# Rebuilding the routing and the row fetch of a second expert layer: one table at the end against one token tile at a time

## The chip, the cores and the metric

The kernel runs on one core of a Trainium2 chip. The metric is the device time in microseconds (us). A core has the matrix engine PE, the vector engine DVE, the scalar engine ACT, GpSimd (POOL) and the sync engine SP, each with its own instruction queue taken in order. They meet through semaphores. DMAs are issued from SP, ACT and POOL.

## The reference, cut to what matters

```python
x = _attn_ref(...)             # (1536, 512) after the heads are laid side by side
x = _moe_ref(x, ...)           # every token through all 8 experts, weighted by P
# second expert layer: each token goes to one expert only
xn = x / (norm(x) + 1e-6); en = emb / (norm(emb) + 1e-6)
logits = xn @ en.T / tau
expert_idx = argmax(logits, axis=1)
probs = softmax(logits); gate_w = probs[arange(N), expert_idx]
for e in range(8):
    mask = expert_idx == e
    h = maximum(x[mask] @ w1[e], 0.0)
    out[mask] = gate_w[mask, None] * (h @ w2[e])
```

Sizes: N = 1536 tokens (12 tiles of 128), D = 512, F = 1024. All is float32. A product is made from high and low parts in float32r: `matmul_x3` issues three PE matmuls for one.

## The kernel before

**Stages.** Attention, then expert layer one (`m1`), then expert layer two (`m2`). Layer one goes through 8 experts; each has three chunks `c` of 512 tokens, and each chunk an up phase (8 groups `f` of 12 matmuls, counted by `m1.up`) and a down phase (32 steps `j` of 3 matmuls, `m1.down`), after which DVE adds the expert's output into `tok` (`m1.y`). In the last expert's last chunk the down phase goes tile by tile (`final`), so that the four y additions come one after another.

**Routing of layer two, before.** The x of 512 tokens is turned by PE (`turn_x`), split by ACT and DVE, multiplied with the split embeddings (`gate`, 512 columns wide) and turned back (`turn_gate`). Chunks 0 and 1 are done inside the last expert of layer one, chunk 2 and everything after it when that expert has ended: norms, argmax and softmax for all 12 tiles at once on DVE, two products for the ranks inside a tile, running sums over tiles and experts, and a place for each token. An expert's tokens fill whole tiles of 128 slots. POOL then writes all twelve tiles of `tok` with twelve indirect DMAs (scatters) to `x_sorted` in DRAM. A row there has 514 columns: x, the weight, the token's number + 1. `x_sorted` is cleared beforehand by 21 DMAs of zeros that SP issues during attention. SP reads the two extra columns back (`meta`), and ACT loads a tile's rows with plain DMAs (`load_row`).

**Layer two, before.** For each expert the engines loop over its tiles `i` (`tile_range`, loop bounds from `start_i`). PE: two up halves `c` of 12 matmuls with a turn of the relu's output between them (`turn_h`), the turn of the next tile's rows (`turn_row(i + 1)`), then the down phase of 24 matmuls with a second `turn_h`. ACT writes y of the tile before (`y_tile`) and high parts; DVE does relu and low parts. POOL stores a tile's y with an indirect DMA (`store`), waits until it has landed, and frees `y_row`.

**Weights of layer two, before.** One raw buffer each for w1 and w2, two sets of split buffers (`w1_p`, `w2_p`). ACT makes the high parts of expert e + 2 when expert e is through (`w1_hi2`, `w2_hi2`), DVE the low part of w1 (`w1_lo2`) and half of w2's (`w2_lo2`), POOL the other half of w2's. SP starts a load of 2 MB when the raw buffer has been split.

## Time and profile before

| | us |
|---|---|
| median of 3 runs | 1652.41 (1651.46 to 1652.56) |
| profiled execution, its own time | 1649.05 |
| its span, first to last instruction | 1647.3 |
| PE busy in the span | 1569.6 (95%) |
| DVE, ACT, POOL busy | 609.7, 469.7, 324.4 |
| mean granted clock of PE, share of full speed | 0.978 |

Busy PE is not PE at its peak: matmuls are pipelined, and the time between the starts of two is less than the duration listed for one. Idle time of another engine costs something only where PE, or the end, waits for it. The page's slices show PE at 9 tenths or more through layer one, a hollow at the layer change, and 9 again after it. The profile's line numbers (L391 to L393 are the three matmuls of `matmul_x3`) are those of the functions printed above.

### The profile page before, as it was taken

How to read it: one execution, taken by the hardware profiler on the slowest of the kernel's cores; microseconds unless marked ns; L12 is line 12 of the kernel's file. 1: busy time of each engine (PE TensorE's matmuls, PEld its weight loads, DVE VectorE, ACT ScalarE, POOL GpSimd, SP SyncE). 2: the span in 40 equal slices, each digit the busy share in tenths (PEclk: the TensorE clock that was granted, in tenths of full speed). 3: DMA queues.
4: the chain of work that ended last, by engine and by line, in shares of the span. 5: the costliest groups of instructions: out<-in, count | busy, mean ns of one | idle time of the engine just before them, and what ended most of it. 6: DMA issues, size and time to landing. Idle time of an engine off the chain costs nothing.

```text
span 1647.3 us, 21247 instructions
## 1 busy us (share of the span) xinstructions
PE 1569.6 (95%) x7516; PEld 1309.9 (80%) x7517; DVE 609.7 (37%) x1021; ACT 469.7 (29%) x864; POOL 324.4 (20%) x527
## 2 busy tenths in 40 slices
PE   7999999999999999999999999999999992799998
PEld 6899998788888888888888888888888771577776
DVE  5888888342221211211211322322222234554324
ACT  4777777112111111111111211211111132654113
POOL 4445444100300300210020030030030004332202
PEclk8999999999999999999999999999999995899999
DMA  4665664100100110110110110020020014754310
GB/s 121 177 156 141 157 141 162 52 1 0 69 35 1 62 40 0 51 51 0 51 51 0 51 51 0 0 102 0 0 82 21 0 52 141 262 191 143 132 45 24
DMA packets 50405, 115.94 MB, mean 70 GB/s; under 512 B 7862, under 2 KB 9910, under 8 KB 50368
## 3 DMA queue, kind: packets, MB, share of 16 engines
q1 hardware_dynamic: 44432, 102.39, 20.1%
q10 hardware_dynamic: 3536, 6.75, 1.5%
q0 software_dynamic: 2400, 6.31, 1.0%
q8 instruction: 22, 0.36, 0.1%
q14 instruction: 15, 0.12, 0.0%
HBM read 81.58 MB, written 13.40 MB: 58 GB/s over the span
## 4 chain that ended last, share of the span: by engine, by line
PE 85%; DVE 4%; DMA 3%; issue 3%; POOL 3%; ACT 1%; SPq 1%; DVEq 0%; ACTq 0%; POOLq 0%
PE psum L391 24%; PE psum L393 24%; PE psum L392 24%; PE psum L624 3%; DMA w_raw<-in_moe_w_dram 2%; PE psum L613 2%; PE psum L637 1%; PE psum L638 1%; PE psum L614 1%; PE psum L595 1%; PE psum L829 1%; DVE row_min L1118 1%; PE psum L649 1%; POOL x_sorted L530 1%; DVE pt_lo L1108 1%
## 5 line engine op out<-in xcount | busy, mean ns | idle before, releaser
L976 ACT ACTIVATE h_hi<-psum 128x512 fp32r<-128x512 f32 x192 | 114.9, 599 | 867.5 <-PE psum L393 867.5
L391 PE MATMUL psum<-xt_lo,w_hi 128*128 128x512 f32 x768 | 303.9, 396 | 0.2 <-DVE xt_lo L1213 0.2
L393 PE MATMUL psum<-xt_hi,w_lo 128*128 128x512 f32 x768 | 301.1, 392 | 0.0
L391 PE MATMUL psum<-w_lo,h_hi 128*128 128x512 f32 x768 | 300.0, 391 | 0.0
L393 PE MATMUL psum<-w_hi,h_lo 128*128 128x512 f32 x768 | 299.3, 390 | 0.0
L392 PE MATMUL psum<-w_hi,h_hi 128*128 128x512 f32 x768 | 298.9, 389 | 0.0
L392 PE MATMUL psum<-xt_hi,w_hi 128*128 128x512 f32 x768 | 298.8, 389 | 0.0
L1298 DVE SCALAR_TENSOR_TENSOR h_lo<-psum,h_hi 128x512 fp32r<-128x512 f32 x192 | 132.7, 691 | 360.8 <-ACT h_hi L976 360.7
L424 POOL CAST w_hi<-w_raw 128x512 fp32r<-128x512 f32 x64 | 39.9, 624 | 813.1 <-PE psum L393 803.8
L1341 DVE SCALAR_TENSOR_TENSOR tok<-psum,route,tok 128x512 f32<-128x512 f32 x84 | 57.5, 744 | 384.6 <-PE psum L393 384.6
L393 PEld LDWEIGHTS psum<-xt_hi,w_lo 128*128 128x128 f32 x768 | 144.2, 188 | 33.4
L392 PEld LDWEIGHTS psum<-xt_hi,w_hi 128*128 128x128 f32 x768 | 144.2, 188 | 31.5
L393 PEld LDWEIGHTS psum<-w_hi,h_lo 128*128 128x128 f32 x768 | 144.1, 188 | 30.6
L392 PEld LDWEIGHTS psum<-w_hi,h_hi 128*128 128x128 f32 x768 | 144.2, 188 | 30.3
L391 PEld LDWEIGHTS psum<-xt_lo,w_hi 128*128 128x128 f32 x768 | 144.4, 188 | 29.7 <-DVE xt_lo L1213 0.4
L391 PEld LDWEIGHTS psum<-w_lo,h_hi 128*128 128x128 f32 x768 | 144.2, 188 | 29.9
L1108 DVE TENSOR_TENSOR pt_lo<-psum,pt_hi 128x384 fp32r<-128x384 f32 x192 | 98.1, 552 | 35.8 <-ACT pt_hi L877 33.7
L884 ACT ACTIVATE prob<-psum,row_bias,row_scale 128x768 f32<-128x768 f32 x96 | 96.5, 1006 | 20.3 <-POOL row_bias L468 20.2
L877 ACT CAST pt_hi<-psum 128x384 fp32r<-128x384 f32 x192 | 83.1, 487 | 44.5 <-PE psum L624 44.5
L1118 DVE TENSOR_REDUCE row_min<-psum 128x1 f32<-128x768 f32 x96 | 90.9, 947 | 8.3 <-PE psum L614 8.3
L508 POOL TENSOR_TENSOR w_lo<-w_raw,w_hi 128x512 fp32r<-128x512 f32 x64 | 83.4, 1303 | 12.7 <-issue 7.4
L613 PE MATMUL psum<-k_b,q_b 128*128 128x384 f32 x192 | 75.0, 390 | 8.3 <-DMA q_b<-bits 4.0
(236 smaller groups left out, 1903.5 us busy)
## 6 DMA issues: line engine op xcount, KB each, us to landing
w_raw<-in_moe_w_dram SPq DMA_DIRECT2D x32, 2048.0 KB, 8.3
k_hh<-k_hi SPq DMA_DIRECT2D x32, 192.0 KB, 3.0
x_sorted<-zeros SPq DMA_DIRECT2D x21, 257.0 KB, 3.9
x_row<-x_sorted ACTq DMA_DIRECT2D x19, 256.0 KB
k_raw<-in_k_dram SPq DMA_DIRECT2D x8, 384.0 KB, 3.2
v_raw<-in_v_dram SPq DMA_DIRECT2D x16, 192.0 KB, 3.5
k_b<-k_lo SPq DMA_DIRECT2D x16, 192.0 KB, 3.3
q_raw<-in_q_dram SPq DMA_DIRECT2D x7, 384.0 KB, 3.7
```

The lines of the kernel that those rows point to most:

```text
L391: pe.matmul(acc, a[0], b[1], start=start, stop=False)
L392: pe.matmul(acc, a[0], b[0], start=False, stop=False)
L393: return pe.matmul(acc, a[1], b[0], start=False, stop=stop)
L508: pool.tensor_tensor(w2_s[1][:, f, :], w2_raw[:, f, :], w2_s[0][:, f, :].bitcast(F32), ALU.subtract).then_inc(m1.w2_lo, 1)
L613: pe.matmul(o, q_b[u][:, a], k_b[u][:, b], start=True, stop=False)
L877: act.copy(pt_hi[half][:, 3 * c:3 * c + 3, a:a + P], psum[:, 4 + c, 0:HALF].rearrange("p (j i) -> p j i", j=3)).then_inc((s_hi_a, s_hi_b)[ ...
L884: act.activation(prob[t % 2][:].rearrange("p (c j) i -> p c (j i)", c=2), psum[:, 2 * (t % 2):2 * (t % 2) + 2, 0:HALF], ACT.Exp, bias=row_ ...
L976: act.activation(h_s[0][:, f, :], psum[:, f % 4, :], ACT.Relu).then_inc(m1.h_hi, 1)
L1108: dve.tensor_tensor(pt_lo[half][:, 3 * c:3 * c + 3, a:a + P], psum[:, 4 + c, 0:HALF].rearrange("p (j i) -> p j i", j=3), pt_hi[half][:, 3 ...
L1118: dve.tensor_reduce(row_min[:, c], psum[:, 2 * (t % 2):2 * (t % 2) + 2, 0:HALF], AX.XY, ALU.min).then_inc(s_min, 1)
L1298: dve.scalar_tensor_tensor(h_s[1][:, f, :], psum[:, f % 4, :], 0.0, h_s[0][:, f, :].bitcast(F32), ALU.max, ALU.subtract).then_inc(m1.h_lo, 1)
L1341: dve.scalar_tensor_tensor(tok[:, tile, 0:DM], psum[:, 4 + i, :], route[:, e, tile:tile + 1], tok[:, tile, 0:DM], ALU.mult, ALU.add).then_ ...
```

## The change

**Token tiles.** In the last expert of layer one each token tile t goes through its own routing: PE turns the tile (`turn_token`), ACT copies it and squares the rows (`token`), PE multiplies with the embeddings in plain fp32 (`token_logits`), DVE picks the expert as a one-hot row (`choose`), PE counts the tokens before each one (`token_rank`), DVE makes from the rank a one-hot lane times the token's number and a one-hot cell of expert and block (`find_cell`), PE multiplies the two (`table_part`), and DVE adds the product into a table of (expert, block) by lane (`add_part`). The norm no longer stands ahead of the argmax. Tiles 0 to 3 go beside chunk 1's down phase (`tokens_beside`), 4 to 6 beside chunk 2's up phase, 7 to 10 beside its down phase (`tokens_between`), tile 11 behind it. The gate products, `turn_gate`, the running sums and the 512-wide turns and splits for layer two are gone.

**Rows.** `x_sorted`, its zeros and the twelve scatters are gone. SP stores each tile of `tok` in token order to `x_rows` when it is final, and the softmax weights to `weights`. POOL gathers the rows of a tile with an indirect DMA through the table; the first tile's indices come from a product of their own. In each tile POOL now issues the store, a gather of 128 weights (`p_now`) and the gather of the rows for tile i + 2. ACT's `load_row` is gone.

**Weights.** w1 of experts 0, 1 and 2 is loaded ahead of layer two, the second into the place of the then dead x. w2 has two raw buffers. POOL makes all of w2's low parts and those of w1 for experts 0 and 1; DVE only w1's from expert 2 on. In a tile, the second `turn_h` stands at f = 1, not 2. PE has no extra turns of the identity while it waits for the first rows.

```diff
+        def store_x(t):
+            sp.wait_ge(m1.y, (E - 1) * TT + t + 2)
+            sp.dma_start(x_rows_v[t // IT, :, t % IT, :], tok[:, t, :]).then_inc(s_x_stored, 16)
+
+        for t in range(2 * CT):
+            store_x(t)
+        sp.wait_ge(m1.up, CH * KF * E + 1)
+        sp.wait_ge(m2.w1_in, 16)
+        sp.dma_start(w1_odd_raw[:], m2.wa[1]).then_inc(m2.w1_in, 16)
+        store_x(2 * CT)
         sp.wait_ge(m2.w1_lo, 1)
-        sp.dma_start(w1_raw[:], m2.wa[1]).then_inc(m2.w1_in, 16)
-
-        sp.wait_ge(s_sorted, 16 * TT)
-        sp.dma_start(meta[:, 1:, :], x_sorted[0:SLOTS * P, DM:ROW].rearrange("(i p) c -> p i c", p=P)).then_inc(s_meta, 16)
...
-        sp.dma_start(w2_raw[:], m2.wb[1]).then_inc(m2.w2_in, 16)
-        with sp.Fori(2, E) as e:
-
+        sp.wait_ge(m2.w1_in, 32)
+        sp.dma_start(w1_raw[:], m2.wa[2]).then_inc(m2.w1_in, 16)
+        for t in range(2 * CT + 1, TT):
+            store_x(t)
+        sp.wait_ge(s_x_stored, 16 * TT)
+        sp.wait_ge(s_squares, 2 * CT)
+        sp.wait_ge(m2.w2_in, 16)
+        sp.dma_start(w2_odd_raw[:], m2.wb[1]).then_inc(m2.w2_in, 16)
+        sp.wait_ge(s_p_ready, 1)
+        sp.dma_start(weights_v, per_tok[:, 2, :].rearrange("p (b t) -> p b t", b=B)).then_inc(s_p_stored, 16)
+        sp.wait_ge(m2.w2_lo, KF)
+        sp.wait_ge(m2.w2_in, 32)
+        sp.dma_start(w2_raw[:], m2.wb[2]).then_inc(m2.w2_in, 16)
+        for e in range(3, E):
+            sp.wait_ge(m2.w2_lo, KF * (e - 1))
+            sp.wait_ge(m2.w2_in, 16 * e)
+            sp.dma_start(w2_raw_p[e % 2][:], m2.wb[e]).then_inc(m2.w2_in, 16)
             sp.wait_ge(m2.w1_lo, e)
+            sp.wait_ge(m2.w1_in, 16 * e)
             sp.dma_start(w1_raw[:], m2.wa[e]).then_inc(m2.w1_in, 16)
-            sp.wait_ge(m2.w2_lo, HF * e)
-            sp.wait_ge(s_w2_pool, (KF - HF) * e)
-            sp.dma_start(w2_raw[:], m2.wb[e]).then_inc(m2.w2_in, 16)
...
         def store(i):
 
             pool.wait_ge(s_y2, i + 1)
-            copy(idx_now[:], out_idx[:, bass.ds(i, 1)]).then_inc(s_idx, 1)
+            pool.wait_ge(s_xrow, 16 * i + 32)
+            copy(idx_now[:], tab[:, bass.ds(i, 1), :].rearrange("p i c -> p (i c)")).then_inc(s_idx, 1)
             pool.wait_ge(s_idx, i + 1)
             pool.sem_inc(s_pool_go, 1)
...
-
-        w2_lo2(0, 0)
-        w2_lo2(1, 1)
-        pool.wait_ge(s_meta_ready, 1)
+                gather(p_now[:], weights, idx_now[:, 1:2], s_p)
+                pool.wait_ge(s_xrow_t, i + 2)
+                pool.sem_inc(s_pool_go, 1)
+                gather(x_row[:], x_rows, idx_now[:, 2:3], s_xrow)
+                pool.wait_ge(s_out2, 16 * i + 16)
+                pool.wait_ge(s_p, 16 * i + 16)
+                pool.sem_inc(s_y_free, 1)
+
+        first_w1_lo(0, 0, w1_raw)
+        first_w1_lo(1, 1, w1_odd_raw)
+        w2_lo2(0, 0, w2_raw, range(0, 2))
+        pool.wait_ge(s_x_stored, 16 * TT)
+        pool.wait_ge(s_first_idx, 1)
+        gather(x_row[:], x_rows, first_idx[:], s_xrow)
+        w2_lo2(0, 0, w2_raw, range(2, 5))
+        pool.wait_ge(m2.routed, 1)
+        pool.wait_ge(s_xrow_t, 1)
+        gather(x_row[:], x_rows, tab[:, 1, 1:2], s_xrow)
+        w2_lo2(0, 0, w2_raw, range(5, KF))
+        w2_lo2(1, 1, w2_odd_raw)
+        pool.wait_ge(s_p_stored, 16)
...
+        def turn_token(t, bank):
+            pe.wait_ge(m1.y, (E - 1) * TT + t + 2)
+            if t > 0:
+                pe.wait_ge(s_squares, t)
+            for kd in range(KD):
+                tr = pe.transpose(psum[:, bank, kd * P:kd * P + P], tok[:, t, kd * P:kd * P + P], ident[:])
+            tr.then_inc(s_turned, 1)
+
+        def token_logits(t, bank):
+            pe.wait_ge(s_copied, t + 1)
+            for kd in range(KD):
+                mm = pe.matmul(psum[:, bank, 0:E], x_t[:, kd, :], emb_t[:, kd, :], start=(kd == 0), stop=(kd == KD - 1))
+            mm.then_inc(s_logits, 1)
+
+        def token_rank(t, bank):
+            pe.wait_ge(s_chosen, t + 1)
+            pe.matmul(psum[:, bank, 0:E], prior[:], chosen[:], start=True, stop=False)
+            pe.matmul(psum[:, bank, 0:E], ones[:], counts[:, t % 2, :], start=False, stop=True).then_inc(s_rank, 1)
+
+        def table_part(t, bank):
+            pe.wait_ge(s_cell, t + 1)
+            if t > 0:
+                pe.wait_ge(s_added, t)
+            pe.matmul(psum[0:CELLS, bank, 0:P], cell[:].rearrange("p e r -> p (e r)"), lane_id[:], start=True,
+                      stop=True).then_inc(s_table, 1)
+
+        def tokens_beside(j, n):
+
+            for t in range(CT):
+                if j == 7 * t:
+                    if t == 0:
+                        pe.wait_ge(m1.h_lo, KF * n + 4 + 5)
+                    turn_token(t, 0)
+                if j == 7 * t + 3:
+                    if t == 0:
+                        pe.wait_ge(m1.h_lo, KF * n + 5 + 5)
+                    token_logits(t, 1)
+                if j == 7 * t + 6:
+                    if t == 0:
+                        pe.wait_ge(m1.h_lo, KF * n + 6 + 5)
+                    token_rank(t, 2)
+                if j == 7 * t + 9:
+                    if t == 0:
+                        pe.wait_ge(m1.h_lo, KF * n + 7 + 5)
+                    table_part(t, 3)
...
+        def tokens_between(f, i, n):
+
+            t = 2 * CT - 1 + i
+            if f == 2:
+                turn_token(t, 0)
+            if f == (3 if i == 0 else 1):
+                if i == 0:
+                    pe.wait_ge(m1.h_lo, KF * n + 7 + 5)
+                table_part(t - 1, 3)
+            if f == 4:
+                token_logits(t, 1)
+            if f == 7:
+                token_rank(t, 2)
+
...
-        ones_of = chosen[:].rearrange("p t e -> p (t e)")
-        pe.matmul(psum[:, 5, 0:TT * E], tri[:], ones_of, start=True, stop=True)
-        pe.matmul(psum[:, 6, 0:TT * E], ones[:], ones_of, start=True, stop=True).then_inc(s_rank, 1)
+        table_part(TT - 2, 3)
+        turn_token(TT - 1, 0)
+        token_logits(TT - 1, 1)
+        token_rank(TT - 1, 2)
+        pe.wait_ge(s_total_in, 1)
+        pe.matmul(psum[0:E, 5, 0:1], counts[:, TT % 2, :], ones[:, 0:1], start=True, stop=True).then_inc(s_total, 1)
+        table_part(TT - 1, 3)
+        pe.wait_ge(s_added, TT)
+        pe.matmul(psum[:, 4, 0:1], table[0:CELLS, :], ident[0:CELLS, 0:1], start=True, stop=True).then_inc(s_first, 1)
+        pe.wait_ge(s_begin_in, 1)
+        pe.matmul(psum[0:CELLS, 6, 32:33], earlier[0:E, :], spot[0:E, 5:6], start=True, stop=True)
+        pe.matmul(psum[0:1, 6, 48:48 + E + 1], spot[0:E, 4:5], reach[0:E, :], start=True, stop=True).then_inc(s_begin, 1)
+        pe.wait_ge(s_slot_in, 1)
+        pe.matmul(psum[:, 7, 0:COLS], table[0:CELLS, :], slot_of[0:CELLS, :], start=True, stop=True).then_inc(s_slots, 1)
...
+        def token(t, bank):
+
+            if t > 0:
+                act.wait_ge(s_logits, t)
+            act.wait_ge(s_turned, t + 1)
+            act.copy(x_t[:].rearrange("p k i -> p (k i)"), psum[:, bank, :]).then_inc(s_copied, 1)
+            act.wait_ge(s_copied, t + 1)
+            act.activation(psum[:, bank, :], tok[:, t, :], ACT.Square,
+                           accum_out=per_tok[:, 0, t:t + 1]).then_inc(s_squares, 1)
...
+        def choose(t, bank):
+
+            dve.wait_ge(s_logits, t + 1)
+            scores_, best = psum[:, bank, 0:E], per_tok[:, 4, t:t + 1]
+            link(dve.tensor_reduce(best, scores_, AX.X, ALU.max))
+            link(dve.scalar_tensor_tensor(pick[:], scores_, best, per_exp[:, 3, :], ALU.is_ge, ALU.mult))
+            link(dve.tensor_reduce(spot[:, 0:1], pick[:], AX.X, ALU.max))
+            link(dve.tensor_scalar(chosen[:], pick[:], spot[:, 0:1], None, ALU.is_equal))
+            dve.sem_inc(s_chosen, 1)
+            link(dve.tensor_tensor(counts[:, (t + 1) % 2, :], counts[:, t % 2, :], chosen[:], ALU.add))
+            if t == TT - 1:
+                dve.sem_inc(s_total_in, 1)
+            link(dve.tensor_copy(logit[:, t, :], scores_))
+
+        def find_cell(t, bank):
+
+            dve.wait_ge(s_rank, t + 1)
+            link(dve.tensor_tensor(pick[:], psum[:, bank, 0:E], chosen[:], ALU.mult))
+            link(dve.tensor_reduce(spot[:, 1:2], pick[:], AX.X, ALU.add))
+            link(dve.tensor_scalar(spot[:, 2:3], spot[:, 1:2], -(P / 2 - 0.5), EVEN, ALU.add, ALU.add))
+            link(dve.scalar_tensor_tensor(spot[:, 3:4], spot[:, 2:3], EVEN, spot[:, 1:2], ALU.subtract, ALU.subtract))
+            link(dve.tensor_scalar(lane_id[:], lane[:], spot[:, 3:4], tok_id[:, t:t + 1], ALU.is_equal, ALU.mult))
+            link(dve.scalar_tensor_tensor(cell[:], block_of[:].unsqueeze(1).to_broadcast([P, E, TT]), spot[:, 2:3],
+                                          chosen[:].unsqueeze(2).to_broadcast([P, E, TT]), ALU.is_equal, ALU.mult))
+            dve.sem_inc(s_cell, 1)
+
+        def add_part(t, bank):
+
+            dve.wait_ge(s_table, t + 1)
+            part = psum[0:CELLS, bank, 0:P]
+            if t == 0:
+                link(dve.tensor_copy(table[0:CELLS, :], part))
+            else:
+                link(dve.tensor_tensor(table[0:CELLS, :], table[0:CELLS, :], part, ALU.add))
+            dve.sem_inc(s_added, 1)
...
                     if last and c == CH - 1:
+                        add_part(2 * CT - 2 + i, 3)
+                        choose(2 * CT - 1 + i, 1)
+                        find_cell(2 * CT - 1 + i, 2)
                         dve.wait_ge(*((s_down_tile, i + 1) if i < CT - 1 else (m1.down, n + 2)))
```

POOL's order in layer two after the change: `first_w1_lo` for experts 0 and 1; `w2_lo2(0)` f 0 and 1; gather of tile 0; f 2 to 4; gather of tile 1; f 5 to 7; `w2_lo2(1)`; and then, for each expert e, the loop above and `w2_lo2(e + 2)`.

## Rows read from the trace of the kernel before

**Rows 1.** Timeline of PE and DVE at layer one's end: start, us, engine, line, operation
```profile
1351.48 0.39 PE L393 MATMUL psum<-w_hi,h_lo 128*128 128x512 f32 x1
...
1351.91 0.75 DVE L1341 SCALAR_TENSOR_TENSOR tok<-psum,route,tok 128x512 f32<-128x512 f32 x1 [4.69 <-PE psum L393]
```

**Rows 2.** Windows across the layer change: us, busy times, PEclk, DMA share, GB/s
```profile
1350.00:1372.00 22.00, 9.73 (x53) 5.74 (x51) 14.17 (x58) 11.66 (x25) 2.35 (x6) 0.78 0.01 1
...
1372.00:1409.00 37.00, 11.16 (x31) 8.55 (x32) 10.85 (x18) 9.79 (x15) 20.86 (x20) 0.55 0.61 214
```

**Rows 3.** Timeline of the gap between the layers and of tile 0, all engines
```profile
1363.34 0.26 DVE L1380 TENSOR_TENSOR chosen<-logit,per_tok 128x96 f32<-128x96 f32 x1
...
1368.23 0.16 DVE L1396 TENSOR_TENSOR start<-start 128x5 f32<-128x5 f32 x1
...
1387.93 0.40 ACTq L1019 DMA_DIRECT2D x_row<-x_sorted  x1
...
1391.66 1.09 PE L820 MATMUL psum<-ident,x_row 128*128 128x128 f32 x4 [26.78 <-DMA x_row<-x_sorted]
...
1394.22 0.79 PE L391 MATMUL psum<-w_lo,x_hi 128*128 128x512 f32 x1 [1.48 <-DVE x_lo L1427]
...
1397.37 0.63 PE L392 MATMUL psum<-w_hi,x_hi 128*128 128x512 f32 x1
```

**Rows 4.** PE's group of g_row turns (xcount), then DVE's timeline in layer two
```profile
L829 PE MATMUL psum<-ident,g_row 128*128 128x128 f32 x136 | 22.1, 288 | 17.4 <-DVE g_row L1449 17.4
...
1405.27 0.69 DVE L1449 TENSOR_SCALAR g_row<-psum 128x512 f32<-128x512 f32 x1 [1.11 <-issue]
...
1484.89 0.69 DVE L1449 TENSOR_SCALAR g_row<-psum 128x512 f32<-128x512 f32 x1
...
1516.74 4.63 DVE L1285 TENSOR_TENSOR w_lo<-w_raw,w_hi 128x1024 fp32r<-128x1024 f32 x4 [0.25 <-ACT w_hi L963]
...
1565.28 0.69 DVE L1449 TENSOR_SCALAR g_row<-psum 128x512 f32<-128x512 f32 x1 [5.96 <-PE psum L393]
...
1578.07 0.69 DVE L1449 TENSOR_SCALAR g_row<-psum 128x512 f32<-128x512 f32 x1 [5.96 <-PE psum L393]
...
1610.72 4.63 DVE L1285 TENSOR_TENSOR w_odd_lo<-w_raw,w_odd_hi 128x1024 fp32r<-128x1024 f32 x4 [0.25 <-ACT w_odd_hi L963]
...
1630.15 0.69 DVE L1449 TENSOR_SCALAR g_row<-psum 128x512 f32<-128x512 f32 x1 [5.90 <-PE psum L393]
```

**Rows 5.** PE's waits in layer two: total us, times, longest
```profile
PE psum L829 <- DVE g_row L1449: 17.4, 7, 4.7
```

**Rows 6.** Timeline of PE: a small fp32 product, and four turns, inside a stream
```profile
316.60 0.36 PE L731 MATMUL psum<-g,ones 128*128 128x96 f32 x2
...
317.06 0.39 PE L392 MATMUL psum<-w_hi,h_hi 128*128 128x512 f32 x1
...
1266.35 0.60 PE L692 MATMUL psum<-ident,tok 128*128 128x128 f32 x4
...
1267.02 0.40 PE L392 MATMUL psum<-xt_hi,w_hi 128*128 128x512 f32 x1
```

**Rows 7.** POOL and SP timelines in layer two; landing times: one store, all stores, scatters
```profile
1403.80 5.20 POOL L536 TENSOR_TENSOR w_odd_lo<-w_raw,w_odd_hi 128x512 fp32r<-128x512 f32 x4 [13.05 <-ACT w_odd_hi L968]
...
1410.02 1.01 POOL L545 DMA_INDIRECT out_dram<-y_row,idx_now  x1 [0.90 <-POOL idx_now L424]
...
1483.51 6.21 POOL L536 TENSOR_TENSOR w_odd_lo<-w_raw,w_odd_hi 128x512 fp32r<-128x512 f32 x4 [9.40 <-ACT w_odd_hi L968]
...
1409.13 0.38 SPq L387 DMA_DIRECT2D w_raw<-in_moe_w_dram  x1
...
DMA to landing us min/median/max: 7.1/7.1/7.1
...
DMA to landing us min/median/max: 2.3/2.8/8.0
...
DMA to landing us min/median/max: 3.1/3.4/3.9
```

More of the change, by code:

```diff
@@ L745, in expert @@
                         pe.wait_ge(s_emb, 1)
-                    if f == 3 and last and c == 2:
-                        pe.wait_ge(m2.logits, 1)
+                    if last and c == 2 and f in (0, 3):
+                        pe.wait_ge(*((s_squares, CT) if f == 0 else (s_added, CT)))
                     for kd in range(KD):
@@ L981, in expert @@
                         copy_gate(m1, f - 2, 4 + f - 2)
-                    if last and c > 0 and 2 <= f < 2 + KD:
-                        x_t_hi(m2, c - 1, f - 2, 4 + f - 2)
-                        square((c - 1) * CT + f - 2)
+                    if last and c == 2 and f in (1, 3, 5):
+                        token(f // 2 + 4, 4)
+                if last and c == 1:
+                    for t in range(CT):
+                        token(t, 0)
                 if first and c == 0:
@@ L1006, in _ @@
         expert(E - 1, last=True)
[L1007 to L1010 removed]
+        act.wait_ge(m1.down, CH * E + 1)
+        w2_hi2(0, 0, w2_raw)
         act.wait_ge(s_act_in, 3)
         act.activation(per_tok[:, 2, :], per_tok[:, 1, :], ACT.Sqrt).then_inc(s_act_out, 1)
[L1013 to L1019 removed]
         def x_hi(i):
@@ L1312, in expert @@
                             first_y(f - 2)
-                    if last and c == 2 and f == 0:
-                        logits(m2, 0, 3)
-                    if last and c > 0 and 2 <= f < 2 + KD:
-                        x_t_lo(m2, c - 1, f - 2, 4 + f - 2)
+                    if last and c == 2:
+                        if f in (4, 6):
+                            add_part(f // 2 + 2, 7)
+                        if f in (3, 5, 7):
+                            find_cell(f // 2 + 3, 6)
+                        if f in (2, 4, 6):
+                            choose(f // 2 + 3, 5)
+                if last and c == 1:
+                    for t in range(CT):
+                        if t > 0:
+                            add_part(t - 1, 3)
+                        choose(t, 1)
+                        find_cell(t, 2)
+                    add_part(CT - 1, 3)
                 if first and c == 0:
@@ L1325, in expert @@
                     embeddings()
-                if c == CH - 1:
-                    if last:
-                        w1_lo2(0, 0)
-                    else:
-                        w1_lo(e + 1)
+                if c == CH - 1 and not last:
+                    w1_lo(e + 1)
                 if not (last and c == CH - 1):
@@ L1344, in expert @@
                     gate_weights()
+                if last and c == 0:
+                    route_tables()
         dve.sem_inc(m1.h_lo, 4)
```

394 lines of the change are left out of this document (190 added, 204 removed).

## The prediction

> **What bounds the kernel now.** I read the page first (PE busy 95% of the span, so it is PE's order and its gaps that matter), then the windows around the layer change, PE's waits, and the timelines of each engine there. The first expert layer runs PE without a gap at clock 1.00 until 1351.7 (its last 512-wide matmul starts at 1351.48, and they follow each other at 0.23) [rows 1]. The second layer's first matmul starts at 1394.22: a gap of 42.5 us in which PE does only small work. In it the windows show the granted clock at a mean of 0.78 and then 0.55: mostly the lower of its two levels, 1.2 GHz, once PE has had little to do [rows 2]. What fills the gap is a chain on other engines [rows 3]: routing in small DVE operations, then twelve scatters on POOL, the read of the first rows from 1387.93, turning and splitting them from 1391.66.
>
> Then come 17 tiles (136 turns of g_row, eight in a tile) [rows 4]. In the long expert a tile's first relu repeats every 12.79 us (1565.28, 1578.07). Sixteen intervals of that are 204.6 us, while the first and the last stand 224.9 apart (1405.27, 1630.15): 20.3 us are lost, most of it early (the first five, to 1484.89, take 79.6 where 64.0 would do) [rows 4]. The DVE rows that split w1 for a coming expert stand between the relu rows so that the experts are seen to have 1, 1, 1, 2, 3, 7, 1, 1 tiles (the 7 lie between the two such rows shown). With one tile to an expert, loading and splitting 4 MB sets the pace. PE waits 17.4 us for the relu in this stage [rows 5], behind weight splits on DVE, and each wait costs clock too.
>
> **The change, part by part.** T is the end of layer one's last matmul, t0 the start of layer two's first.
>
> *1. Routing by tile, on PE, in the last expert.* Four turns (one pass each) delay the stream by 0.44 (0.67 from the turn to the second matmul, less 0.23); one plain fp32 product is two passes and delays it by 0.23 (0.46 less 0.23), though it has only 96 columns [rows 6]. So a pass costs some 0.09 to 0.11 however narrow. A token tile now needs 4 turns, 4 logit products (8 passes), 2 rank products (4) and one table product (2): 18 passes. Before T stand eleven turns, logits and ranks and ten tables: 11 x 16 + 10 x 2 = 196 passes, 17.6 to 21.6 us; I take 20.5, as most stand in separate insertions. Removed from that stretch: eight groups of turns at 0.44 (3.5), eight 512-wide gate matmuls at 0.23 (1.9), four small turns (0.5): 5.9.
> The Trainium skill (TensorE: Matmul & The Clock Gate, LDWEIGHTS) has a weight load take its columns / 1.2 ns, 107 ns for 128, however few columns are multiplied. By that alone the passes would cost an estimated 21.0; the rows agree to within their spread.
>
> New waits: in the last down phase, token_rank(t-1) is issued ahead of a round's last triple (f = 7), and table_part(t-1) ahead of the triple f = 1 of the next round. From the rank's start DVE needs 0.35 + 0.2 latency + six operations. Small ones take 0.16 and 96-wide ones 0.26 [rows 3], with 0.03 between, so 1.5 to 1.7. PE arrives after 0.4 for the rank and two triples of 0.7. That is a stall of about 0.5 in three of the four rounds, 1.5 in all; nothing else is queued on PE behind it but the same stream. Beside the second down phase and the third up phase, DVE's 2.2 per slot (h_lo 0.69 and six operations) fits in PE's 2.75 plus insertions: zero. T moves by 20.5 - 5.9 + 1.5 = 16.1, to 1367.8 (bounds 10 and 22).
>
> *2. From T to the first matmul.* find_cell(10) and the last y (0.75 [rows 1]) end at T + 1.7; four turns to 2.3; the copy on ACT (0.6) to 2.95; logits to 3.9; four DVE operations to 4.7; ranks to 5.3; six operations to 6.7; table product, addition, the one-column product and the index to 8.0; POOL starts the gather at 8.3, 0.3 of issue included. The stored x rows are home at 1.8 + 3.9 (as the slowest of the twelve scatters landed in 3.9), and SP then starts w2 of expert 1 at 5.9. Alone such an indirect DMA of 256 KB lands in about 3, issued with a weight load in 7.1 to 8.0 [rows 7]. So the rows land at 11.4 at best; I take 15.0, the time at which the load's 2 MB are nearly home (a median load takes some 9). Turn, copy and split take 2.6, as from 1391.66 to 1394.22 [rows 3]: t0 = T + 17.6 = 1385.4, that is 8.8 before the old one. No turns of the identity keep PE awake in that gap; the same low clock as before meets tile 0 (a matmul that took 0.39 takes 0.63 in tile 0 [rows 3]; thirteen of them came before the clock rose, 0.2 each: 2.6). The scatters, the zero fill of x_sorted, the meta read and the gate pieces after T all go; the fills ran beside attention, where the page's chain does not name them and PE runs on, so I take zero for them.
>
> *3. Tile 0.* DVE no longer splits weights of expert 1 between x_lo(0) and the relu. The first relu comes at t0 + 2.8 + 2.6 = 1390.8 instead of 1405.27: 14.5 ahead.
>
> *4. POOL becomes a server.* It now splits all of w2's low half: 8 pieces, twice the 5.20 of four [rows 7], W = 10.4. (Before, DVE did four of them.) Per tile it does S: the index copy, the y store 1.1 later, then two gathers 1.3 apart (1.0 and 0.3 of issue each), and then it waits for the store and the weight column to land before it frees y_row. The x rows for tile i+2 are thus issued 3.6 after S(i) starts. SP issues the next w2 load exactly when W ends, which is when S begins, as it is now, the load at 1409.13 and the store at 1410.02 [rows 7]. So the store takes some 7.3 again and S holds POOL 8.7; the x gather, behind the store in the same queue, lands at about S + 10.3. Behind S on POOL is the next W, and PE waits for both: PE's turn_row(i+2) stands in mid tile i+1, 5.6 after its start, and 7.2 of that tile follow it. A cycle for a one-tile expert is 10.4 + 8.7 = 19.1, against 12.8 of PE work and against 17.1, 18.9, 17.1 between relus today.
> Working it through from t0: W(1) ends at 14.1 (f5 to 7 start after the second gather), x(2) lands at 24.4, wanted at 21.0. Tile 2 starts at 24.4 + 7.2 + 2.0 (low clock after the stall) = 33.6. S(1) at 33.3, x(3) 43.6, tile 3 at 52.8; S(2) at 52.5, tile 4 at 72.0; S(3) at 71.7, tile 5 at 91.2. Its relu: t0 + 94.0 = 1479.4, against 1484.89: of the 14.5 ahead only 5.5 remain. That is the core of the forecast.
>
> *5. The rest.* Eleven intervals: 140.7, plus 5.4 for one more such stall behind W(5) and its clock, against 145.3 today. With two or more tiles to an expert S fits easily (its gather lands at tile start + 10, wanted at 18). DVE's splitting of w2 before a relu goes, which is why I count no other loss at the experts' borders. The second w2_raw buffer and the early loads of w1 take DMA off the path. The turn at f = 1 instead of 2: its relu is done by then, zero. The tail, y, store and landing, is as now. The last relu: 1479.4 + 146.1 = 1625.5 against 1630.15.
>
> Sum: -4.7 us on a span of 1647.3, which is one execution of 1649.05; the runs' median is 1652.41, and the difference is carried to it: **1647.7, say 1647.**
>
> **The rivals.** *A, the forecast:* POOL sets the pace through the one-tile experts, and what was won in the gap is mostly spent. 45%, its own range 1641 to 1653.
>
> *B, the gathers land fast.* If stores and gathers land in 2.9 as in the quiet long expert, S is 5.1 and x lands at S + 6.5: the cycle is 15.6, the first rows come 3.6 sooner, tile 2 is not held, tile 5 starts at t0 + 75, and the fifth interval's stall goes. -4.7 - 3.6 - 16.2 - 4 = about -29, 1623; halfway cases give 1635. For it: the w2 loads now have two raw buffers and spread out. Against it: each of the stores issued within 1 us of a weight load today took over 7 [rows 7]. 30%.
> The Trainium skill (DMA: Bandwidth & Descriptors, Anatomy of one DMA) gives such a POOL-issued DMA 2.0 us + bytes / 436e3, 2.6 for 256 KB; taken alone it is this case. The 7.1 shown disagrees with it while weights are moving.
>
> *C, slower.* POOL's pieces stretch. Where DVE works beside them, four take up to 6.2 instead of 5.2 [rows 7]; W is then 12.4, and with S at 9.7 the cycle 22.1. Four cycles more by 3.0 each are +12, so 1660. It decides from a cycle of 20.5 on, or from passes over 0.13 us. For it: five early weight splits of DVE now meet a POOL that never rests. Against: in the one-tile stage the four took about 5.2 each time. 25%.
>
> *D:* the gap shortens but T moves by as much: included in A's upper end.
>
> **Range and chances.** B's far end and C's give 1622 and 1661; a tenth is left out on each side at 1624 and 1660. A measurement of this kernel tells about 0.2%, 3.3 us, from no change: faster means under 1649.1. B gives 0.30, seven tenths of A 0.31: faster 0.61. The rest of A's upper end and a little of C: same 0.18. C: slower 0.21.
>
> **What the new profile should show.** Layer one's last matmul near 1368 with PE at clock 1.00 up to it; the first second-layer matmul near 1385; the DVE relu of tile 0 near 1391; PE waits named x_row, some 3 to 7 us each, in tiles 1 to 4, ending when an indirect gather lands; store and gather landings of 7 and more beside weight loads; relu intervals of 12.8 from tile 6 on. The forecast is wrong if T moves by over 22 (chains of choose and find_cell that PE waits for in every round), if turn_row hardly waits (B), or if W takes over 12 (C).

## The result, and the profile after

The changed kernel takes 1675.76 us (median of 4 runs, 1674.48 to 1676.21) against 1652.49 beside it on the same chip (1651.46 to 1654.18): a ratio of 1.0139, 95% interval 1.0121 to 1.0156. It is slower by 23 us where 5 less were forecast, and it lies outside the range of 1624 to 1660. The profiled execution has a span of 1673.9, 26.6 more than before, and a mean granted clock of 0.977.

The windows over the end of layer one and the start of layer two (busy times with counts in the order PE, PEld, DVE, ACT, POOL; then granted clock, DMA share, GB/s), to be held against [rows 2]:

```profile
1255.00:1340.00 85.00, 85.00 (x432) 71.01 (x430) 31.66 (x105) 17.92 (x36) 0.00 (x0) 1.00 0.07 25
1340.00:1375.00 35.00, 26.12 (x115) 20.97 (x116) 20.35 (x44) 9.29 (x14) 14.03 (x6) 0.84 0.37 135
1375.00:1410.00 35.00, 20.87 (x104) 16.76 (x103) 20.22 (x58) 9.64 (x20) 12.22 (x8) 0.74 0.24 83
1410.00:1440.00 30.00, 18.68 (x70) 14.66 (x69) 22.87 (x18) 13.67 (x22) 18.25 (x17) 0.69 0.36 107
```

PE is full with POOL idle until 1340. Then POOL begins to work, and PE is busy for 26 of 35 us in what was to be a dense stream; the clock, 1.00 until then, falls to 0.84 and 0.74 before layer one has ended. Its waits from 1255 on (total, times, longest):

```profile
PE psum L954 <- DVE g_row L1589: 14.2, 3, 9.7
PE psum L945 <- DMA x_row<-x_rows,idx_now: 14.1, 5, 7.2
PE psum L814 <- DVEq L1428: 12.3, 6, 6.1
PE psum L938 <- DVEq L1550: 5.0, 1, 5.0
```

L954 are the turns of the relu's output and L945 those of the gathered rows. Before, PE waited 17.4 for the relu in seven waits [rows 5]. Now a single one is 9.7 long, and two new kinds stand in the routing: `table_part` (L814) waits for `find_cell`, and the last product (L938) for `slot_of`. The timelines of DVE and POOL show why. First in the last up phase, beside `find_cell` of tile 6:

```profile
1344.93 2.12 DVE L1424 SCALAR_TENSOR_TENSOR spot<-spot 128x1 f32<-128x1 f32 x1
1347.08 2.33 DVE L1425 TENSOR_SCALAR lane_id<-lane,spot,tok_id 128x128 f32<-128x128 bf16 x1
1349.45 2.29 DVE L1426 SCALAR_TENSOR_TENSOR cell<-block_of,spot,chosen 128x96 f32<-128x96 f32 x1
...
1361.99 0.75 DVE L1514 SCALAR_TENSOR_TENSOR tok<-psum,route,tok 128x512 f32<-128x512 f32 x1
...
1372.60 0.75 DVE L1514 SCALAR_TENSOR_TENSOR tok<-psum,route,tok 128x512 f32<-128x512 f32 x1
...
1391.45 0.75 DVE L1514 SCALAR_TENSOR_TENSOR tok<-psum,route,tok 128x512 f32<-128x512 f32 x1
```
```profile
1344.66 9.30 POOL L568 TENSOR_TENSOR w_lo<-w_raw,w_hi 128x1024 fp32r<-128x1024 f32 x4 [109.04 <-ACT w_hi L1091]
```

A piece is one low-part subtraction on POOL. The same three operations take 0.16, 0.35 and 0.32 where POOL is idle. Each now ends with a POOL piece of 2.33 (9.30 / 4): three operations, three pieces. The cell comes 6.1 late, and PE has nothing else to do. The y additions stand 10.6, 10.8 and 8.0 apart instead of 4.8 to 5.4; the last is at 1391.45, against 1351.91 [rows 1].

Then DVE and POOL from the routing to the first relu, with the issue of the next weight load on SP:

```profile
1402.69 4.66 DVE L1549 TENSOR_SCALAR slot_of<-slot,begin_col 96x21 f32<-96x21 f32 x1
...
1411.21 0.69 DVE L1577 TENSOR_TENSOR x_lo<-psum,x_hi 128x512 fp32r<-128x512 f32 x1
...
1412.99 12.84 DVE L1583 TENSOR_SCALAR per_tok<-per_tok 128x12 f32<-128x12 f32 x1
...
1428.27 0.69 DVE L1589 TENSOR_SCALAR g_row<-psum 128x512 f32<-128x512 f32 x1 [2.18 <-issue]
...
1654.04 0.69 DVE L1589 TENSOR_SCALAR g_row<-psum 128x512 f32<-128x512 f32 x1 [6.27 <-PE psum L427]
```
```profile
1402.27 1.29 POOL L579 DMA_INDIRECT x_row<-x_rows,first_idx  x1 [4.84 <-DVE first_idx L1538]
1403.60 3.70 POOL L575 TENSOR_TENSOR w_lo<-w_raw,w_hi 128x512 fp32r<-128x512 f32 x3
1411.23 0.96 POOL L579 DMA_INDIRECT x_row<-x_rows,tab  x1 [3.93 <-PE psum L945]
1412.22 3.77 POOL L575 TENSOR_TENSOR w_lo<-w_raw,w_hi 128x512 fp32r<-128x512 f32 x3
1415.95 9.85 POOL L575 TENSOR_TENSOR w_odd_lo<-w_odd_raw,w_odd_hi 128x512 fp32r<-128x512 f32 x8
...
1450.01 0.18 POOL L458 COPY idx_now<-tab 128x3 uint32 x1
...
1459.27 12.00 POOL L575 TENSOR_TENSOR w_odd_lo<-w_raw_odd,w_odd_hi 128x512 fp32r<-128x512 f32 x8 [3.38 <-DMA p_now<-weights,idx_now]
1471.22 1.18 POOL L458 COPY idx_now<-tab 128x3 uint32 x1
```
```profile
1426.65 0.41 SPq L414 DMA_DIRECT2D w_raw<-in_moe_w_dram  x1
```

An addition to twelve columns, 0.17 otherwise, takes 12.84: it starts 0.8 after POOL's row of eleven pieces and ends with it, at 1425.8. The relu of tile 0 is behind it in DVE's queue and comes at 1428.27, though layer two's first matmul started at 1412.04. On SP the store of the softmax weights (1426.18) and, queued behind it, a load of 2 MB (1426.65) wait as long. POOL's cycle for a one-tile expert, from one index copy to the next, is 21.2 here (1450.01 to 1471.22), and 19.5 and 20.1 in the cycles beside it; the first five intervals between relus take 84.8 (to 1513.10) against 79.6, the later ones of the long expert 12.47 against 12.79, and the whole stage from first to last relu takes 225.8 against 224.9 [rows 4].

One more difference stands far from all edits, in layer one, whose code is the same. DVE's h_lo, one for each up group of 12 matmuls:

```profile
706.14 0.69 DVE L1461 SCALAR_TENSOR_TENSOR h_lo<-psum,h_hi 128x512 fp32r<-128x512 f32 x1 [2.11 <-ACT h_hi L1104]
708.94 0.69 DVE L1461 SCALAR_TENSOR_TENSOR h_lo<-psum,h_hi 128x512 fp32r<-128x512 f32 x1 [2.11 <-ACT h_hi L1104]
```

And in the kernel before:

```profile
706.02 0.69 DVE L1298 SCALAR_TENSOR_TENSOR h_lo<-psum,h_hi 128x512 fp32r<-128x512 f32 x1 [2.05 <-ACT h_hi L976]
708.77 0.69 DVE L1298 SCALAR_TENSOR_TENSOR h_lo<-psum,h_hi 128x512 fp32r<-128x512 f32 x1 [2.06 <-ACT h_hi L976]
```

They stand 2.80 apart now, and 2.745 before (the third is at 711.74 and at 711.51). A chunk, from its first h_lo to the next chunk's, takes 44.17 instead of 43.80; 24 of them are 8.8 us.

### The profile page after: what moved, and what is told of

The parts are those of the page before. It is cut to its first block, busy times and chain, and to the rows that moved or that the text cites. A ratio compares the mean times of both kernels' runs of the same rounds, so it can differ in the third digit from the quotient of the medians.

```text
span 1673.9 us, 21630 instructions
## 1 busy us (share of the span) xinstructions
PE 1594.4 (95%) x7654; PEld 1332.3 (80%) x7655; DVE 627.6 (37%) x1094; ACT 469.1 (28%) x861; POOL 407.0 (24%) x594
## 4 chain that ended last, share of the span: by engine, by line
PE 83%; DVE 5%; POOL 4%; issue 3%; DMA 2%; ACT 1%; POOLq 0%; DVEq 0%; ACTq 0%
PE psum L425 23%; PE psum L427 23%; PE psum L426 23%; PE psum L685 3%; PE psum L674 2%; PE psum L698 1%; PE psum L699 1%; PE psum L675 1%; DMA p_now<-weights,idx_now 1%; PE psum L656 1%; POOL w_odd_lo L575 1%; DVE row_min L1241 1%; PE psum L710 1%; DMA x_row<-x_rows,idx_now 1%; POOL w_lo L575 1%
## 5 line engine op out<-in xcount | busy, mean ns | idle before, releaser
L425 PE MATMUL psum<-w_lo,h_hi 128*128 128x512 f32 x768 | 304.1, 396 | 0.0
L426 PE MATMUL psum<-xt_hi,w_hi 128*128 128x512 f32 x768 | 303.2, 395 | 0.0
L685 PE MATMUL psum<-ident,prob 128*128 128x128 f32 x576 | 79.9, 274 | 1.0 <-DVE pt_lo L1231 0.8
```

What stands on the lines that cost most here:

```text
L425: pe.matmul(acc, a[0], b[1], start=start, stop=False)
L426: pe.matmul(acc, a[0], b[0], start=False, stop=False)
L685: tr = pe.transpose(psum[:, 4 + c, j * P:j * P + P], prob[par][:, 3 * c + j, :], ident[:])
```

## The experiments

All ratios are to the kernel before, run beside each on the same chip. The experiments ran on four chips, where the median of the kernel before was 1650.8 to 1653.8, so differences in us between two versions are good to some 2 us. L numbers in an experiment's rows are its own and lie a few lines off.

**1. POOL's first w1 pieces go to DVE.**
```diff
-        first_w1_lo(0, 0, w1_raw)          # on POOL
-        first_w1_lo(1, 1, w1_odd_raw)
...
                         add_part(2 * CT - 2 + i, 3)
+                        first_w1_lo(i // 2, i % 2)   # on DVE, two of the eight pieces in a round
                         choose(2 * CT - 1 + i, 1)
```


> The changed kernel, with the low parts of w1 of experts 0 and 1 made by DVE (two pieces of 1.16 us in each of the four rounds of the last down phase) and no longer by POOL (ten pieces' worth, 18.8 us of POOL time between 1344 and 1382). Theory: while one of these POOL pieces (2.36 us each) runs, a small DVE operation in SBUF is held until the piece ends, as at 1344.93 (2.12), 1347.08 (2.33), 1349.45 (2.29), 1366.43 (1.98), 1368.56 (2.18), 1379.38 (2.20). Without them the waits of PE for the cell (12.3 us in six) fall to about 2, the clock stays near 1.00 in the last down phase, the rounds take 7 to 8 us instead of 10.7, layer one's last matmul ends near 1379 instead of 1391, and the time falls by 10 to 13 us, to about 1664. Rival: the passes of PE and its waits for the copy and the squares on ACT set the rounds; then the held operations disappear but the rounds stay over 10 us and the time falls by under 3. Second rival: DVE's own pieces, 2.3 us a round, stand in front of choose and hold PE as long as the POOL pieces did.

Measured: 1668.23 us, ratio 1.0096 (1.0075 to 1.0116), so 7 us less than the change. The wait for the cell and the y additions:

```profile
PE psum L812 <- DVEq L1426: 3.2, 5, 1.6
```
```profile
1361.93 0.75 DVE L1522 SCALAR_TENSOR_TENSOR tok<-psum,route,tok 128x512 f32<-128x512 f32 x1
...
1363.02 2.36 DVE L1454 TENSOR_TENSOR w_odd_lo<-w_odd_raw,w_odd_hi 128x1024 fp32r<-128x1024 f32 x2
...
1369.90 0.75 DVE L1522 SCALAR_TENSOR_TENSOR tok<-psum,route,tok 128x512 f32<-128x512 f32 x1
```
```profile
1346.00:1377.00 31.00, 29.93 (x162) 23.85 (x160) 22.25 (x65) 11.42 (x19) 0.00 (x0) 1.00 0.41 157
```

Rounds of 8.0, DVE's two pieces in the gap before `choose`, the wait down from 12.3 to 3.2, and the granted clock at 1.00 through the last down phase. From the last expert's first y to its last there are 113.9 us, against 128.6 in the changed kernel and 93.6 in the kernel before: 14.6 of the delay were POOL's pieces. Its profile has the first relu 13.5 earlier than the changed kernel's (1414.73 against 1428.27) but the last only 10.1: the rest went in the one-tile experts, where PE's wait for gathered rows grew from 14.1 to 19.1. `slot_of` (5.0 still) and the 12-column addition were held as before.

**2. POOL waits for the softmax weights.**
```diff
+        pool.wait_ge(s_p_ready, 1)
         w2_lo2(0, 0, w2_raw, range(5, KF))
```


> The changed kernel, with POOL waiting for the softmax weights before it makes the last three low pieces of w2 of expert 0 and all eight of expert 1. Theory: the 128x12 tensor_scalar at 1412.99 took 12.84 us because eleven POOL pieces stood back to back from 1412.22 to 1425.80; with nothing on POOL it takes under 0.3, the weights are ready near 1413.6, the first relu comes at 1415 instead of 1428.27, and the weights' store and the load of w2 of expert 2, queued behind it on SP, leave 9 to 12 us earlier. What reaches the end is less, if POOL sets the pace: its first store follows the eighth piece at about 1427.2 instead of 1430.47, so the whole of layer two moves by 3 to 5 us, and the time is about 1671.5. Rival: the late relu is on the path, and the 13 us reach the end, 1663. Second rival: POOL starts 1.5 us later and nothing is won, 1675 to 1677.

Measured: 1677.97, ratio 1.0157 (1.0136 to 1.0179): nothing won, as the second rival had it. DVE and POOL:

```profile
1413.38 0.17 DVE L1584 TENSOR_SCALAR per_tok<-per_tok 128x12 f32<-128x12 f32 x1
...
1417.34 0.69 DVE L1590 TENSOR_SCALAR g_row<-psum 128x512 f32<-128x512 f32 x1 [3.52 <-PE psum L427]
...
1423.67 8.11 DVE L1449 TENSOR_TENSOR w_lo<-w_raw,w_hi 128x1024 fp32r<-128x1024 f32 x4 [0.26 <-ACT w_hi L1092]
```
```profile
1417.70 13.01 POOL L575 TENSOR_TENSOR w_odd_lo<-w_odd_raw,w_odd_hi 128x512 fp32r<-128x512 f32 x8
1430.65 1.18 POOL L458 COPY idx_now<-tab 128x3 uint32 x1
```

The addition is back at 0.17 and the relu comes 11 earlier. But DVE then reaches its w1 pieces while POOL still makes w2's: DVE's four take 8.11 instead of 4.63, POOL's eight 13.01 instead of 9.85, and POOL's first index copy, which leads its first store, starts at 1430.65, as it did at 1430.47. The wait moves from the relu (14.2 to 1.4) to the gathered rows (14.1 to 26.8). POOL sets the pace, and what counts is the pieces of both engines together, since they hold each other up.

**3. Half of w2's low parts back on DVE**, from expert 1 on, each engine counting on a semaphore of its own.
```diff
-        w2_lo2(1, 1, w2_odd_raw)
+        w2_lo2(1, 1, w2_odd_raw, range(HF, KF))      # POOL; DVE makes f 0 to 3 behind s_p_ready
...
-                w2_lo2(2 * e2 + u + 2, u, w2_raw_p[u])
+                w2_lo2(2 * e2 + u + 2, u, w2_raw_p[u], range(HF, KF))
...
                 w1_lo2(e + 2, u)                      # DVE
+                w2_lo2(e + 2, u, w2_raw_p[u])
```


> The changed kernel, with the low parts f 0 to 3 of w2 made by DVE from expert 1 on, and only f 4 to 7 by POOL. Theory (POOL sets the pace of the one-tile experts): POOL's stretch of an expert falls from 10 to 13 us to about 5.5, its cycle from 20.5 to 15, so PE no longer waits for the gathered rows (14.1 us in five now, under 3 then); over four cycles 12 to 18 us, less what DVE's 2.4 us a time costs ahead of the relu (up to 2 in each of four experts) and less the 12.8 us hold on the softmax weights, which shrinks as POOL has seven pieces in a row and not eleven. Time about 1663 to 1667. Rival: the two engines lock each other out, so that the sum of their pieces stays what it is, and the waits only move from the rows to the relu: 1673 to 1677.

Measured: 1658.88, ratio 1.0028 (1.0016 to 1.0040): 17 us less than the change, more than expected.

```profile
1415.06 7.96 DVE L1593 TENSOR_SCALAR per_tok<-per_tok 128x12 f32<-128x12 f32 x1
```
```profile
1414.28 3.78 POOL L578 TENSOR_TENSOR w_lo<-w_raw,w_hi 128x512 fp32r<-128x512 f32 x3
1418.01 4.97 POOL L578 TENSOR_TENSOR w_odd_lo<-w_odd_raw,w_odd_hi 128x512 fp32r<-128x512 f32 x4
...
1446.19 0.19 POOL L461 COPY idx_now<-tab 128x3 uint32 x1
...
1461.45 0.18 POOL L461 COPY idx_now<-tab 128x3 uint32 x1
```

POOL's cycle is 15.3 (1446.19 to 1461.45), as expected, and no wait for gathered rows is left among PE's waits; the relu has 13.9 in seven. The row of POOL pieces behind the addition is now seven long, and it is held 7.96, again to the row's end (1422.98).

**4. The three together.** The diffs of experiments 1, 2 and 3 in one kernel. 

> The first-weights pieces on DVE, POOL held until the softmax weights are ready, and w2's low parts halved, all three in the changed kernel. Theory: the first gives its 7.7 us again, and once POOL's stretch is short the hold on the softmax weights, which alone gave nothing, gives some 3 to 6 more on top of the halved w2: about 1653 to 1657. Rival: they overlap, and the sum is that of the first and the halved w2 alone, 1658 or more.

Measured: 1636.53, ratio 0.9892 (0.9865 to 0.9919). It is 39 us below the changed kernel and 17 below the kernel before, where the three gains alone sum to about 22; the expectation was at least 17 too high. Against experiment 3 the last y comes 15.9 earlier (1376.68 against 1392.61), which is the part of experiment 1, and now all of it reaches the end. The hold on the softmax weights adds a few us: the first relu stands 8.3 behind layer two's first matmul instead of 11.8. No run has experiments 1 and 3 without 2, so this split is read from traces and not tested.

**5. No POOL piece beside the routing**, on top of those three.
```diff
-        w2_lo2(0, 0, w2_raw, range(0, 2))
...
         gather(x_row[:], x_rows, first_idx[:], s_xrow)
-        w2_lo2(0, 0, w2_raw, range(2, 5))
         pool.wait_ge(m2.routed, 1)
+        w2_lo2(0, 0, w2_raw, range(0, 5))
```


> As the run before in this list, and POOL makes no low part of w2 of expert 0 until the routing is done: pieces 0 to 4 follow m2.routed instead of standing beside the routing chain. Theory: the 96x21 tensor_scalar that took 4.66 us takes under 0.3 and the two operations held beside tile 11 (0.57 and 1.08) take 0.4, so the routing is ready 5 us sooner; the first rows then set t0, which comes 1 to 2 us sooner; but eight pieces (10 us) then stand between the first gather and tile 0's down phase, which starts 7 us after t0, so 1 to 3 us are given back. The time is within 2 us of the run before. Rival: with the routing ready sooner the second gather leaves sooner and 4 to 5 us are won.

Measured: 1636.61, ratio 0.9885 (0.9858 to 0.9912), the same. PE no longer waits 5.0 for `slot_of` but 2.3 for the first rows and 5.2 for x_lo: the norm chain ahead of x_lo is held instead.

```profile
1390.50 1.03 DVE L1585 TENSOR_TENSOR per_tok<-per_tok 128x12 f32<-128x12 f32 x1
1391.57 1.19 DVE L1586 TENSOR_TENSOR per_tok<-per_tok 128x12 f32<-128x12 f32 x1
1392.79 1.19 DVE L1587 TENSOR_SCALAR per_tok<-per_tok 128x12 f32<-128x12 f32 x1
```
```profile
1390.24 6.17 POOL L578 TENSOR_TENSOR w_lo<-w_raw,w_hi 128x512 fp32r<-128x512 f32 x5 [1.40 <-DVEq L1581]
```

Here each held operation gets in behind one piece of 1.23, and so do two later ones (1.01 and 1.20), beside pieces of the very size that held the addition for 12.84.

**6 and 7. 32 bytes**, in the kernel before and in the changed one.
```diff
     tok = place("tok", [P, TT, ROW], F32)
+    top[0] += 32
```


> The kernel before, with 32 unused bytes per partition behind tok, so that the turned x, the raw and split weights and the h buffers all start at a multiple of 64 bytes, as in the changed kernel, instead of 32 over one. Nothing is computed differently. Theory: the up groups of layer one took 2.80 us in the changed kernel and 2.745 in the kernel before, from the place of the operands in SBUF alone; then the up groups here take 2.80, a chunk takes 44.17 instead of 43.82, and the time rises by 7 to 8 us, to 1660, less what layer two's tiles gain (12.46 instead of 12.79 between relus, up to 5). Rival: the 0.055 us come from something else (the larger program, other queues), and the time stays within 1 us of 1652.5.

 

> The changed kernel, with the same 32 bytes behind tok, so that its operands start 32 over a multiple of 64 bytes as in the kernel before. Theory of the place in SBUF: up groups of 2.745, chunks of 43.82, layer one's last matmul about 8 us earlier, the time near 1668 (more if the tiles of layer two go back from 12.46 to 12.79). Rival: nothing moves, 1675 to 1677.

Measured: 1653.35 (0.9998, 0.9988 to 1.0008) and 1679.75 (1.0160, 1.0138 to 1.0181). Up groups stay at 2.745 in the one and at 2.80 in the other. So it is not the remainder of 64 bytes that decides.

**8 and 9. 256 bytes.** In the changed kernel, 96 bytes behind `tok` and 64 ahead of the split weights; then the 64 alone.
```diff
     tok = place("tok", [P, TT, DM], F32)
+    top[0] += 96       # in the first of the two
...
+    top[0] += 64
     shared = top[0]
```


> The changed kernel, with 96 unused bytes behind tok and 64 more ahead of the split weights, so that the turned x, the raw weights, the split weights and h all start at the same remainder of 256 bytes as in the kernel before (a shift by 32 had changed nothing). Theory of the place in SBUF: the up groups of layer one go from 2.80 to 2.745. Rival: they stay at 2.80, and the place, at this grain, is not the reason.

 

> The changed kernel, with 64 unused bytes ahead of the split weights and nothing moved behind tok. The run with both shifts had brought the up groups of layer one from 2.80 to 2.745, with turned x at remainder 224 and w1 at 160 of 256 bytes; here x stays at 128 and w1 comes to 64. Theory: it is the distance of the two operands that PE reads at once (x 64 over w1, remainder of 256, in every quick kernel so far, 128 in every slow one): 2.745. Rival: it is the place of x alone (224 and 0 quick, 128 and 160 slow): 2.80.

Measured, one run each: 1669.90 and 1668.71. The last one's h_lo rows:

```profile
704.42 0.69 DVE L1462 SCALAR_TENSOR_TENSOR h_lo<-psum,h_hi 128x512 fp32r<-128x512 f32 x1 [2.05 <-ACT h_hi L1105]
707.17 0.69 DVE L1462 SCALAR_TENSOR_TENSOR h_lo<-psum,h_hi 128x512 fp32r<-128x512 f32 x1 [2.06 <-ACT h_hi L1105]
```

2.745 in both, so the place in SBUF is the cause after all, at least for this step. It is not that of x alone, which experiment 9 left where it was. In all fourteen kernels the distance between turned x and w1 (remainder of 256) goes with the rate: x is 64 bytes over w1 in every kernel with 2.745, and 128 in every one with 2.80. Both shifts changed w1's own place too; with five remainders of w1 seen, that w1's place alone decides is not excluded. The change had made `tok` 96 bytes shorter and the tables between x and w1 2240 bytes longer, and so moved one against the other.

**10. The turn alone, in the kernel before.**
```diff
-                    if f == 2:
+                    if f == 1:
                         turn_h(i, 1)
```


> The kernel before, with the second turn of g_row at f = 1 instead of f = 2 in the down phase, as in the changed kernel, and nothing else. Theory: the split of the turned rows is then ready before f = 4, where the kernel before loses 0.18 to the wait and 0.15 more to the next start in each tile; relus of the long expert stand 12.46 apart instead of 12.79, and 17 tiles give 5.5 us: 1647 to 1649. Rival: my prediction's: the move costs and gives nothing, 1652.5 to 1654.

Measured: 1640.90, ratio 0.9920 (0.9901 to 0.9940). Two relus of the long expert:

```profile
1587.84 0.69 DVE L1449 TENSOR_SCALAR g_row<-psum 128x512 f32<-128x512 f32 x1 [6.40 <-PE psum L393]
...
1600.33 0.69 DVE L1449 TENSOR_SCALAR g_row<-psum 128x512 f32<-128x512 f32 x1 [6.39 <-PE psum L393]
```

12.49 against 12.79 [rows 4], and 219.6 between the first and the last relu instead of 224.9: the 5.3 us of the theory. The time fell by 12, though; the profiled execution, the slowest of its four runs, by 4, and in it layer one's column sums stand 1.15 later (317.75 against 316.60), in a stretch with the same code. What the rest of the 12 is, no profile here shows.

**11 and 12. All of it.** The three edits, both shifts, and POOL's first five pieces behind `slot_of`; then those five cut into two and, once the norm chain is done, three, with DVE's half of expert 1 behind expert 0's tile.
```diff
         gather(x_row[:], x_rows, first_idx[:], s_xrow)
+        pool.wait_ge(s_slot_in, 1)
+        w2_lo2(0, 0, w2_raw, range(0, 2))      # the first of the two versions: range(0, 5)
+        pool.wait_ge(s_act_in, 4)              # second version only
+        w2_lo2(0, 0, w2_raw, range(2, 5))      # second version only
         pool.wait_ge(m2.routed, 1)
```


> The three edits together, the shift by 96 and 64 bytes, and POOL's first five pieces of w2 of expert 0 moved behind the slot_of operation (two of them stood beside tile 11's choose, three beside slot_of). Theory: the three edits gave 1636.5; the up groups give back 0.055 in each of 192, 8 us with the down groups; slot_of, on the way to the first turn of x since the rows now land before it, takes under 0.3 instead of 4.65 and gives 2 to 3. About 1626. Rival: the five pieces hold the softmax chain ahead of x_lo, as when nothing stood beside the routing, and the last part gives nothing: 1629.

 

> The version that took 1629.3, with two changes of place. POOL makes two pieces of w2 of expert 0 behind slot_of and the next three only when DVE's norm chain is done; and DVE makes its half of w2 of expert 1 behind expert 0's tile and not ahead of its relu. Theory (what holds DVE is the length of POOL's unbroken row of pieces): the 128x12 tensor_tensor that took 4.60 us is held under 1, x_lo comes at x_hi's end, 1385.8 instead of 1389.23, and the first layer-two matmul 3.5 sooner; the first relu is no longer behind 6.83 us of pieces, which gives 4.8 more there and costs up to 2.5 ahead of the next relu. Together 4 to 6: 1624 to 1626. Rival: loading and splitting the one-tile experts' weights paces the stage by now, and the gain is under 2.

Measured: 1629.34, ratio 0.9856 (0.9836 to 0.9876), and 1627.71, ratio 0.9842 (0.9817 to 0.9868). In the first of them:

```profile
1380.70 0.23 DVE L1570 TENSOR_SCALAR slot_of<-slot,begin_col 96x21 f32<-96x21 f32 x1
...
1383.23 4.60 DVE L1588 TENSOR_TENSOR per_tok<-per_tok 128x12 f32<-128x12 f32 x1
```
```profile
1381.61 6.19 POOL L580 TENSOR_TENSOR w_lo<-w_raw,w_hi 128x512 fp32r<-128x512 f32 x5
```

Against the three together the last y comes 7.5 earlier (1369.14 against 1376.68) and the time is 7 lower, which fits the shifts' 8.8 in layer one. `slot_of` is free, and an operation soon behind it pays, as the rival had it. In the second, with a row of two pieces, the same operation takes 0.90 and the first relu comes 5.1 earlier, but the median only 1.6: its rival holds too. The relu still costs 10.6 in six waits.

## Why the prediction failed, step by step

Predicted and real last relu are 1625.5 and 1654.04, 28.5 apart: 23.4 in T (0.2 ahead of the last y at 1391.45, as in [rows 1], so 1391.2 against 1367.8), 3.2 from T to t0, 10.8 from t0 to the first relu, and -8.9 in the stage after it. Of the 23.4, 14.6 are POOL's pieces (experiment 1), 4.2 the rest of the last expert, and 4.6 lie ahead of it. The tail behind the last relu, taken "as now", is 2.7 longer.

- **Step 1 failed, and with it the forecast.** Its passes were nearly right: in experiment 1 eight logit passes put the next matmul off by 0.90, 0.11 each, the top of its range. With POOL out of the way the last expert is 20.3 longer than before (113.9 less 93.6), where 16.1 were summed; rounds take 8.0 rather than the 7.3 that the sum implies. Its stalls were not: "a stall of about 0.5 in three of the four rounds" and "zero" beside the up phase came from DVE durations read where POOL was idle, and POOL's w1 pieces, which the change puts into just these rounds, were costed nowhere. They are 14.6 us in T (experiment 1). The sentence that T over 22 would break the forecast, through chains that PE waits for, named the place but no cause.
- **Not in the sum at all:** the place of two operands in SBUF, 8.8 us in layer one (experiments 8, 9); the sum took unchanged code for unchanged time. About 3 us came back ahead of layer one: its column sums stand at 313.77 instead of 316.60 [rows 6]. The removed fills, taken at zero, are not shown to be the reason, since experiment 6 still has them:

```profile
314.60 0.36 PE L732 MATMUL psum<-g,ones 128*128 128x96 f32 x2
```

  The traces of the changed kernel's versions have 313.69 to 315.19 there, and those of the kernel before 314.60 to 317.75.
- **Step 2** was near: 20.8 from T to t0, 17.6 forecast. But it was `slot_of`, held from within the gather's issue to the end of three POOL pieces (4.66), and not the landing of the rows, that set it. The gather was issued at T + 11.1 where 8.3 was forecast, and landed in 3.6; with `slot_of` free the first rows are turned 3.75 after the issue (experiment 11). So the value of 15.0 rested on the wrong bound.
- **Step 3 failed:** the first relu "at t0 + 2.8 + 2.6" came at t0 + 16.2, behind an addition held for 12.84.
- **Step 4** had the mechanism and its terms: POOL as server, S of 8.7 measured at 9.3, W of 10.4 measured at 9.9 to 12.0, cycle 19.1 measured at up to 21.2. Beside the weight loads stores landed in 5.1 to 6.9 and rows in 3.9 to 7.4, nearer the forecast's 7.3 than rival B's 2.9; the median of 3.6 over all rows comes from the quiet long expert. Tile 5's relu stands at t0 + 101.1 where 94.0 was forecast. Experiment 3 puts the price of POOL's share of w2 at 17 us.
- **Step 5** was too dear, 140.9 from there to the last relu where 146.1 was forecast: the turn at f = 1, put at zero, gives 0.3 a tile, 5.3 in all (experiment 10). This is part of what kept the miss from being larger.
- **Rival C** was the one that came true in sign and kind ("POOL's pieces stretch"), with 25%; its cycle of 22.1 came near the 21.2 measured, and its price, 12 us, was read from the pieces of POOL alone. Small DVE operations held behind them, and PE and its clock behind those, cost more.

The Trainium skill (SBUF — State Buffer, Who interferes with whom) says that DVE and GpSimd share one pair of ports under an exclusive lock, taken for a whole instruction, by a DVE operation with two SBUF inputs or in a 2-port mode (which tensor_scalar can enter). The rows above agree: the held ones read and write SBUF, while those that read PSUM (x_lo 0.69, the copy 0.17) were not held. By that rule alone an operation waits for the piece in front of it, 1.24 or 2.33, as in experiment 5; the 12.84 span eleven of them, and there the measurement decides.

## What to carry to other kernels

Before giving GpSimd bulk work on SBUF, list the small VectorE operations that will run beside it, and ask who waits for each: a 0.17 us step can come back as one GpSimd piece or as the length of its unbroken row, and it costs most in a chain that TensorE waits for. Keep such rows short, above all behind an indirect DMA on GpSimd, or put them where VectorE reads PSUM. Where both engines have bulk work in SBUF, reckon with the sum of their times. After any edit of the SBUF layout compare the rate of the matmuls that were not edited; 64 bytes of padding were worth 7 us here.
